# One multiplication by zeros fewer and a small load on another queue, at the start of a fused attention and MLP kernel

## What is computed

```python
scores = scale * np.matmul(q, k.transpose(0, 1, 3, 2))
thresh = np.max(scores, axis=-1, keepdims=True) - tau
scores = np.where(scores >= thresh, scores, -1000000000.0)
scores = scores - np.max(scores, axis=-1, keepdims=True)
attn = np.exp(scores)
attn = attn / (np.sum(attn, axis=-1, keepdims=True) + 1e-09)
x = np.matmul(attn, v)                      # heads side by side: (4, 576, 512)
...
h = np.maximum(xt @ w_tok1, 0.0) @ w_tok2   # over tokens
u = x + h.transpose(0, 2, 1)
x = u + np.maximum(u @ w_ch1, 0.0) @ w_ch2  # over channels
...
h = np.maximum(x @ w_in, 0.0)
gate = 1.0 / (1.0 + np.exp(-conv_out))      # conv_out: 3 taps along the sequence of h
out = h * gate @ w_out
```

## Time and profile before

| | us |
|---|---|
| median of 3 runs | 848.66 |
| lowest and highest | 848.38, 848.97 |
| the profiled execution | 847.75 |
| its span, first to last instruction | 845.9 |
| TensorE busy | 822.6 (97%) |
| VectorE busy | 417.8 (49%) |
| ScalarE busy | 413.0 (49%) |
| mean granted TensorE clock | 0.997 |

### The profile page before, as it was taken

The page is one execution under the profiler, slowest core; times in us unless marked ns, Lnnn a source line. Parts: engine busy times, 40 slices in busy tenths (PEclk is TensorE's granted clock), DMA queues, the critical chain, the costliest instruction groups (busy, mean ns, idle before and its releaser), DMA issues.

```text
span 845.9 us, 15190 instructions
## 1 busy us (share of the span) xinstructions
PE 822.6 (97%) x5656; PEld 669.8 (79%) x5656; DVE 417.8 (49%) x829; ACT 413.0 (49%) x914; POOL 257.8 (30%) x202
## 2 busy tenths in 40 slices
PE   8989999999999998899999999999999999999998
PEld 4657777777677767788888888888899999898996
DVE  6887877878878784401211211211214819155380
ACT  4878888878878884211211211211114737365461
POOL 0261223223323224460200200110391726428170
PEclk9999999999999999999999999999999999999999
DMA  9311111111111204000000000000320010100101
GB/s 265 112 47 48 48 48 46 46 46 46 46 46 46 63 2 150 1 1 0 1 1 1 0 1 1 1 0 1 137 63 2 1 51 1 50 13 0 50 0 62
DMA packets 20906, 32.70 MB, mean 39 GB/s; under 512 B 4416, under 2 KB 11136, under 8 KB 20864
## 3 DMA queue, kind: packets, MB, share of 16 engines
q1 hardware_dynamic: 20864, 32.13, 11.7%
HBM read 27.41 MB, written 4.72 MB: 38 GB/s over the span
## 4 chain that ended last, share of the span: by engine, by line
PE 87%; ACT 6%; DVE 3%; issue 3%; POOL 0%; ACTq 0%; DVEq 0%; POOLq 0%
PE score L1236 17%; PE score L1351 12%; PE score L1032 6%; PE out_t L1251 4%; PE turn_y L1251 4%; PE mixed L1251 4%; PE turn_x L1251 4%; PE out_t L1127 4%; PE out_t L1336 4%; PE mixed L1127 4%; PE mixed L1179 3%; PE turn_y L1336 3%; PE mixed L1336 3%; PE turn_x L1336 3%; PE turn_x L1058 3%
## 5 line engine op out<-in xcount | busy, mean ns | idle before, releaser
L954 DVE SCALAR_TENSOR_TENSOR h<-score,h 128x512 fp32r<-128x512 f32 (+1 forms) x60 | 38.3, 638 | 243.5 <-ACT h L726 243.5
L726 ACT ACTIVATE h<-score 128x512 fp32r<-128x512 f32 (+1 forms) x60 | 33.3, 555 | 250.4 <-PE score L1236 250.4
L874 DVE TENSOR_SCALAR_CACHE_REDUCE negs<-score,neg_scale 128x576 f32<-128x576 f32 x144 | 112.7, 816 | 60.9 <-PE score L1032 45.6
L891 DVE SCALAR_TENSOR_TENSOR prob<-negs,thresh,exps 128x576 f32<-128x576 f32 x144 | 129.2, 930 | 0.3 <-ACT thresh L627 0.3
L624 ACT ACTIVATE exps<-negs,neg_max 128x576 f32<-128x576 f32 x144 | 104.7, 772 | 2.3 <-DVE negs L874 1.9
L1032 PE MATMUL score<-qk 64*128 64x288 f32 x512 | 86.7, 437 | 1.9 <-DVE negs L874 1.4
L1236 PE MATMUL score<-uh,w1l 128*128 128x512 f32 (+1 forms) x240 | 86.8, 368 | 0.0
L1236 PE MATMUL score<-uh,w1h 128*128 128x512 f32 (+1 forms) x240 | 86.8, 368 | 0.0
L1236 PE MATMUL score<-ul,w1h 128*128 128x512 f32 (+1 forms) x240 | 86.8, 368 | 0.0
L592 POOL TENSOR_TENSOR zl<-z,zh 128x512 fp32r<-128x512 f32 x32 | 54.2, 1694 | 98.7 <-ACT zh_t L812 98.7
L1032 PEld LDWEIGHTS score<-qk 64*128 64x128 f32 x512 | 47.9, 188 | 28.1 <-issue 13.6
(11 more groups left out here) (184 smaller groups left out, 1967.2 us busy)
## 6 DMA issues: line engine op xcount, KB each, us to landing
qk<-in_qk SPq DMA_DIRECT2D x16, 640.0 KB, 3.9
vm<-in_v SPq DMA_DIRECT2D x16, 320.0 KB, 4.2
result<-ostage SPq DMA_DIRECT2D x16, 256.0 KB, 2.1
w1f<-in_moe_w_ch SPq DMA_DIRECT2D x4, 768.0 KB, 10.9
w2f<-in_moe_w_ch SPq DMA_DIRECT2D x4, 768.0 KB, 7.4
wif<-in_moe_w_in SPq DMA_DIRECT2D x1, 2048.0 KB, 7.8
wof<-in_moe_w_out SPq DMA_DIRECT2D x8, 256.0 KB, 2.6
wt2f<-in_moe_w_tok SPq DMA_DIRECT2D x1, 576.0 KB, 9.4
```

Of the source, the lines that this page charges most:

```text
L874: nc.vector.tensor_scalar(negs[:, i, h, :].rearrange("p (c s) -> p c s", c=2), raw_of[h], neg_scale[:, 0:1], None, ALU.mult, ALU.min, accu ...
L891: nc.vector.scalar_tensor_tensor(out=prob[:, i, h * S:(h + 1) * S], in0=negs[:, i, h, :], scalar=thresh[:, i, h:h + 1], in1=exps[i][:, h, ...
L954: nc.vector.scalar_tensor_tensor(out=h3[:, n % RING, 1, 0:w], in0=hidden_banks[n % 4][:, 0:w], scalar=0.0, in1=h3[:, n % RING, 0, 0:w].bit ...
```

## The change

TensorE's first call becomes `keep_busy(1)`. The load of tau leaves SP's list and is issued by ScalarE on its own queue, ahead of everything else ScalarE does. ScalarE's table load and small activation no longer wait for `tau_used`; that wait stands behind them, ahead of the first exponential.

```diff
             load_qk(0, 0)
-            sp.dma_start(tau_in[:, :], tau.broadcast_to([P, 1])).then_inc(tau_loaded, DMA)
             load_qk(1, 1)
...
         def _(act):
+            nc.scalar.dma_start(tau_in[:, :], tau.broadcast_to([P, 1])).then_inc(tau_loaded, DMA)
             act.wait_ge(cleared, 2)
+            nc.scalar.activation(warm[:, :], ones[:, :], ACT.Exp)
             act.wait_ge(tau_used, 2)
-            nc.scalar.activation(warm[:, :], ones[:, :], ACT.Exp)
...
             pe.wait_ge(zeros_set, 1)
-            keep_busy(2)
+            keep_busy(1)
             for i in range(2):
                 scores((0, 0, i))
                 keep_busy(1)
```

## The result

The changed kernel takes 850.83 us (median of 8 runs), that of before 847.89 (8 runs with the three shown above): a ratio of 1.0030, 95% interval 1.0021 to 1.0039. The change makes the kernel slower by about 2.9 us. A second set on one chip gives 1.0034 (1.0021 to 1.0047). I had forecast 847.6 us: 1 us faster than 848.66, the median of the three runs I had then, which the eight runs put at 847.89.

A forecast was written before the change was run, and what follows sets the result against it. The prediction took the start's chain of engine work, TensorE busy 97%, as the bound. A gain of 1.49 us less 0.5 for shared DMA engines, 0.99, from 848.66 gave 847.67; it predicted 847.6, range 846.6 to 849.1.

The forecast's parts named there:

- What bounds the kernel, and the reading of the chain: Whole span: TensorE is busy 97%, the chain is engine work alone, so time saved at the start is passed on once.
- The base: Starting time for the forecast: 848.66 us, the median of the runs of before, from which the gain is subtracted.
- Zeros A halved, TensorE ready at 4.13: First zeros on TensorE: two instructions fewer save 1.71 us, so TensorE is ready for scores A at 4.13.
- Tau's landing: Tau's load at the start: issued at about 0.75, it lands at 6.15, or 3.7 to 4.7; costs at most 0.09 us.
- The table load: ScalarE at the start: 1.28 us plus 0.20 for the activation move to about 1.2 to 2.7 us and cost nothing.
- Across two queues I take a smaller share, 0.5 us: Load of qk, pair 0: tau's pieces beside it delay it 0.5 us, between bounds of 0 and 2.3.
- If the clock rises at the same 8.06: TensorE at zeros B: clock goes from lower to higher level at 8.06 as before, so zeros B end at about 8.6.
- TensorE stands still and its clock stays low: Rival at the start: qk lands at 6.65, TensorE idles and its clock rises late; +2.3 us, 851.0, chance 0.06.
- load on time, clock late: Rival at the start: the clock rises only past scores B, +0.98 against -0.99 to -1.49; 848.1 to 848.7, chance 0.13.
- more than 1.7 us: Rival near 62.7 to 66.0 us: the clock dip falls away; with the forecast's 0.99 gain 2.0, time 846.7, chance 0.14.

The follow-up runs named there:

- e9: Changed kernel with two later TensorE pauses, near 59 and 315 us, filled by products of the unit matrix: 848.43 us, ratio 1.0009 to before.
- e10: Kernel of before with both later TensorE pauses filled by products of the unit matrix: 846.59 us, ratio 0.9984 to before.
- e3: Kernel of before with only ScalarE's table load and small activation moved ahead of the wait for tau's products: 847.68 us, ratio 0.9999.
- e1: Kernel of before with only tau's load moved to ScalarE's queue, zeros A still two: 848.38 us against 847.82, ratio 1.0008.
- e6: Changed kernel with ScalarE's load reading 128 neighbouring weights instead of tau's one number 128 times; one run, no time given, qk landing after 4.7 us.
- e5: Changed kernel with tau loaded first on SyncE's queue, ahead of qk of pair 0: 849.26 us against 848.26 of before, ratio 1.0012.
- e4: Changed kernel with tau loaded as a single number and spread to 128 partitions by a TensorE product: 847.59 us, ratio 0.9995 to before.
- e11: e4 with both later TensorE pauses filled by products of the unit matrix: 846.74 us, ratio 0.9984 to before.
- e2: Kernel of before with only zeros A cut to one multiplication, tau still second on SyncE's queue: 848.08 us against 847.82, ratio 1.0002.
- e8: Kernel of before with TensorE multiplying the unit matrix by itself in its pauses near 58 and 60 us: 846.94 us against 848.26, ratio 0.9988.

## Why the prediction was wrong

**What bounds the kernel, and the reading of the chain:** right. The first microseconds are passed on: in e9 and e10 the difference at `negs` B (11.81 and 10.55) is 1.26, and that of the spans 845.8 less 844.4, 1.4.

**The base:** 848.66 was high by 0.77, so the forecast gain of 0.99 would have been 846.9. **Zeros A halved, TensorE ready at 4.13:** right (4.21). **Tau's landing:** right within the bounds, 5.74 against 6.15; its share in the path, nothing. **The table load:** right, shown by e3.

**"Across two queues I take a smaller share, 0.5 us":** this step failed. The share was 2.1 us of a bound of 2.3 (qk landing 5.7 after its issue in place of 3.6), in the changed kernel and in e1 alike. I put the value near the lower bound because qk's pieces keep the DMA engines busy; rows 9, with 46 GB/s while tau's pieces were served, had spoken for the other end, and 62 GB/s from 1 to 4 us in the changed kernel bear them out. Of the 2.1, about 1.0 is the single address (e6, one profile); e5 shows that tau ahead on the same queue harms qk less than tau beside it. The Trainium skill's rule (DMA: Bandwidth & Descriptors, section "Issuing engines are not separate DMA queues") speaks for a share above nothing, and does not say how large. e1 agrees with it, 5.7 us for 3.6, and adds that the second queue can cost more than the 0.45 us of issue that it saves.

**"If the clock rises at the same 8.06":** this failed too. Zeros B ran at the lower clock until past 10 us, and were over at 10.73 where I had 8.6. The single zeros A are enough for a later rise: in e4 and e11, with qk on time and no pause, zeros B are slow up to 9.00. e5 prices the late clock without any delay of scores A: 0.72 us at `negs` B against the profile of before, which is itself a late one.

**The rival "TensorE stands still and its clock stays low"** had a chance of 0.06 and 851.0 us (measured 850.83). It had the mechanism, but the close number is in part luck: it starts from 848.66, and its terms of 0.98 and 0.55 us for slow scores B and zeros C did not occur (1.24 and 1.12 us). Its 2.3 us are 0.84 at `negs` B in the profile. In "load on time, clock late" the late clock is what e2, e4 and e11 show, yet scores B lasted 1.71, 1.30 and 1.92, where it counted on 2.22.

**The two parts together** are worse than their sum. One part each costs 0.56 (e1) and 0.26 us (e2), neither clear of its measurement, and together 2.9. With the double zeros a late qk finds the clock up (e1). With the single zeros and qk on time the clock is late, but the start is 1.1 to 1.4 us sooner and pays for it (e2, e4). With both, nothing is saved and the clock is late.

**Where the 2.9 us are.** 1.84 with the later falls gone (e9 less e10). The profiles show 1.26 of it at `negs` B for that pair, and 1.24 between the means of the four profiles of each start (11.95 and 10.71). A still later rise in some executions would fit the rest and the 847.66 to 849.67 us of e9; the four profiles of the changed kernel have none, but e5 and e11 have scores B of 1.90 and 1.92. The remaining 1.1 lies between medians in different groups of mean clock; of the means' 2.4, e9 and e10 account for 1.9. Whether the changed kernel meets the falls near 62 and 318 us more often is open.

**The rival "more than 1.7 us",** that a fall of the clock may vanish, had about the right price (e8 gains 1.3, e10 1.0 us). The change did not bring it. Work in the pauses does; without it the falls come and go, and 2 of 85 runs of before have a mean clock of 1.000.

## What to carry to other kernels

Multiplications by zeros in the chain are not waste to be cut by their length: ask what the engine does in that time if they go, and whether it then runs the next work at half the clock. A tiny broadcast load costs its pieces, not its bytes; beside the load that the kernel waits for it delayed that by 2 us, so keep it behind, or load one number and spread it on chip. And before a difference of 0.3% is explained from two profiles, compare runs at the same mean granted clock and profile each start more than once.

## What the runs showed of the hardware

- 128 pieces of 4 bytes on a second queue delayed the landing of a load of 0.66 MB from 3.6 to 5.7 us after its issue (e1, changed); to 4.7 with distinct addresses (e6).
- TensorE's clock was up when zeros B began in five of five profiles with two multiplications of zeros at the start, and in none of nine with one, whether a pause followed or not.
- A fall of the granted clock to 0.50 followed a stretch in which TensorE was busy 1.87 of 3.20 us, and did not with 3.20 of 3.20. With 2.55 of 3.80 it came in one execution and not in another. About 7 short products more at one place and 4 at another made the kernel 0.16% faster than before (e10).
- The mean granted clock of a run, 0.994 to 1.000, goes with 850.2 to 846.9 us for one and the same kernel: more than the change was expected to bring.
